# The end of a Fourier transform reordered, two column folds and two low halves moved from GpSimd to VectorE

## The reference

```python
scores = scale * q @ k.T + bias          # causal window of 128, one slope per head
x = softmax(scores) @ v                  # -> (4, 576, 512)
mixed = real(fft(fft(x, axis=1), axis=2))
u = x + mixed
un = (u - mean(u)) / sqrt(var(u) + 1e-6)
x2 = u + relu(un @ w_ch1) @ w_ch2        # 512 -> 2048 -> 512
# gate: one of 8 experts per token, sticky along the sequence
out = p[e] * (relu(x2 @ w1[e]) @ w2[e])  # 512 -> 1024 -> 512
```

## Time and profile before

| | |
|---|---|
| median of 3 runs | 922.79 us |
| lowest, highest | 921.07, 926.31 us |
| profiled execution, its own time | 928.07 us |
| its span, first to last instruction | 926.1 us |
| mean granted TensorE clock | 0.975 of full speed |
| busy: PE, DVE, ACT, POOL | 862.1, 459.1, 316.4, 279.7 us |

### The profile page before, as it was taken

The page is one execution under the profiler, slowest core; times in us unless marked ns, Lnnn a source line. Parts: engine busy times, 40 slices in busy tenths (PEclk is TensorE's granted clock), DMA queues, the critical chain, the costliest instruction groups (busy, mean ns, idle before and its releaser), DMA issues.

```text
span 926.1 us, 22607 instructions
## 1 busy us (share of the span) xinstructions
PE 862.1 (93%) x9091; PEld 623.7 (67%) x9092; DVE 459.1 (50%) x851; ACT 316.4 (34%) x469; POOL 279.7 (30%) x293
## 2 busy tenths in 40 slices
PE   8989897698999999999999999947999999999995
PEld 4767676575676767677777777626767777777773
DVE  6999887557333333342424243748994885000000
ACT  5888886345212111111111111111333333333331
POOL 0467777511020101010101000002444444443332
PEclk9999999899999999999999999968999999999998
DMA  8465533345110101011010102513774773111110
GB/s 285 133 175 173 167 113 108 91 132 183 36 46 23 45 23 45 31 36 44 24 45 24 44 8 67 176 48 95 235 238 153 232 233 115 45 42 45 45 34 0
DMA packets 55608, 88.87 MB, mean 96 GB/s; under 512 B 7148, under 2 KB 26171, under 8 KB 55557
## 3 DMA queue, kind: packets, MB, share of 16 engines
q1 hardware_dynamic: 50117, 72.16, 25.4%
q0 software_dynamic: 5440, 16.00, 5.6%
HBM read 70.80 MB, written 16.55 MB: 94 GB/s over the span
## 4 chain that ended last, share of the span: by engine, by line
PE 72%; DVE 7%; DMA 7%; issue 4%; POOL 3%; ACT 3%; SPq 2%; DVEq 0%; POOLq 0%; ACTq 0%
PE psum L920 19%; PE psum L903 19%; PE psum L1084 13%; PE psum L1100 13%; DMA m_mem<-in_qk 3%; DMA arena<-in_mlp_w 1%; DMA m_mem<-x_rows,m_mem 1%; PE psum L1051 1%; PE psum L655 1%; PE psum L864 1%; DVE m_mem L1404 1%; ACT psum L1159 1%; DVE arena L1425 1%; POOL arena L1880 1%; PE psum L872 1%
## 5 line engine op out<-in xcount | busy, mean ns | idle before, releaser
L903 PE MATMUL psum<-m_mem,arena 128*128 (+1 forms) x1728 | 200.4, 274 | 0.0
L920 PE MATMUL psum<-arena,m_mem 128*128 128x512 f16 x864 | 195.3, 379 | 0.0
L903 PEld LDWEIGHTS psum<-m_mem,arena 128*128 128x128 f16 x1728 | 169.2, 98 | 26.5 <-issue 0.2
L920 PEld LDWEIGHTS psum<-arena,m_mem 128*128 128x128 f16 x864 | 84.5, 98 | 90.4
L1084 PEld LDWEIGHTS psum<-m_mem,arena 128*128 x2400 | 137.3, 97 | 6.9 <-issue 1.5
L1084 PE MATMUL psum<-m_mem,arena 128*128 128x128 f16 x2400 | 139.6, 219 | 1.2 <-issue 0.6
L1100 PE MATMUL psum<-arena,m_mem 128*128 x600 | 133.4, 379 | 0.0
L1270 ACT ACTIVATE m_mem<-psum 128x512 f16<-128x512 f32 x72 | 42.9, 596 | 244.1 <-PE psum L903 244.1
L1100 PEld LDWEIGHTS psum<-arena,m_mem 128*128 128x128 f16 x600 | 57.7, 98 | 65.1
L1965 POOL TENSOR_TENSOR arena<-m_mem,arena 128x1024 f16<-128x1024 f32 x9 | 18.0, 1998 | 271.8 <-ACT arena L1285 226.8
L1591 DVE SCALAR_TENSOR_TENSOR m_mem<-psum,m_mem 128x512 f16<-128x512 f32 x72 | 49.7, 691 | 101.3 <-ACT m_mem L1270 101.2
(11 more groups left out here) (242 smaller groups left out, 1081.7 us busy)
## 6 DMA issues: line engine op xcount, KB each, us to landing
dimdft_sb<-in_exp_w SPq DMA_DIRECT2D x74, 256.0 KB, 3.3
wstage<-in_exp_w SPq DMA_DIRECT2D x54, 256.0 KB, 2.9
m_mem<-in_qk SPq DMA_DIRECT2D x16, 576.0 KB, 4.5
arena<-in_v SPq DMA_DIRECT2D x32, 160.0 KB, 2.7
x_rows<-m_mem SPq DMA_DIRECT2D x16, 320.0 KB, 3.0
x_rows<-arena SPq DMA_DIRECT2D x9, 512.0 KB, 2.8
wstage<-in_mlp_w SPq DMA_DIRECT2D x16, 256.0 KB, 3.4
arena<-in_mlp_w SPq DMA_DIRECT2D x16, 256.0 KB, 3.8
```

The costliest lines, as they stand in the source:

```text
L903: last = nc.tensor.matmul(psum[:, 2 + k % 4, (f % 2) * 2 * P:(f % 2 + 1) * 2 * P], w1_sb[:, sp_, c, f * P:(f + 1) * P], unT[:, bass.ds(t % ...
L920: last = nc.tensor.matmul(psum[:, 6 + q, :], hT[:, k % 4, sp_, at:at + P], w2_sb[:, mp, f, :], start=f == 0 and sp_ == 0 and mp == 0, stop ...
```

## The change

It reorders the instruction lists of all five engines around the end of the transform.

- **SyncE** loads rows 0 to 127 of `x_dram` into `xg[:, 0]` itself (new semaphore `xg0_in`) and issues the load of row 288 of each batch right behind it, after weight chunk 8 and a wait for all stores of x; the latter no longer waits for `ulo_done` 8.
- **TensorE**: `spectrum` waits per chunk for the two pairs of that chunk; transpose_un(0) stands after spectrum(3).
- **ScalarE**: x_hi_of for pairs 12 to 15, the first and second middle rows, the last leftover column and the square root get other places.
- **VectorE** takes fold_d(14) and fold_d(15) (`end_fold_d`) and x_lo_of(14) and x_lo_of(15) (`end_x_lo`); middle_lo_of(2) stands before `normalise_u`, unT_lo_of(0) after spectrum_lo(3).
- **GpSimd** keeps folds and low halves up to pair 13 in another order and gathers only `xg[:, 1]` for tile 0, with row numbers straight from `xrow_sb`. `xg_in` counts 16 less from there on.

```diff
@@ SyncE
-            for n in range(WRING + 2, W_TOP + 3):
+            for n in range(WRING + 2, WRING + 5):
+                load_w(n)
+            for par in range(2):
+                sp.wait_ge(x_stored[par], 16 * PAIRS // 2)
+            sp.dma_start(xg[:, 0, :], x_dram[0:P, :]).then_inc(xg0_in, 16)
+            sp.dma_start(x288[0:B, :], ...[HALF]).then_inc(x288_in, 16)
+            for n in range(WRING + 5, W_TOP + 3):
                 load_w(n)
...
-            for par in range(2):
-                sp.wait_ge(x_stored[par], 16 * PAIRS // 2)
-            sp.wait_ge(ulo_done, DH2 * B)
-            sp.dma_start(x288[0:B, :], ...[HALF]).then_inc(x288_in, 16)
             load_w(W_TOP + 3)
@@ TensorE
-                pe.wait_ge(x_split, PPB * b + PPB)
                 for c in chunks:
+                    pe.wait_ge(x_split, PPB * b + 2 * c + 2)
...
             spectrum(2)
-            transpose_un(0, 4, un_first)
             pe.wait_ge(xl_split, B)
             pe.wait_ge(first_copied, 2)
             middle_rows(B)
             spectrum(3)
+            transpose_un(0, 4, un_first)
@@ ScalarE
-            x_hi_of(PAIRS - 4)
...
             spectrum_hi(0, (0,))
+            x_hi_of(PAIRS - 4)
             x_hi_of(PAIRS - 3)
             spectrum_hi(0, (1,))
+            middle_hi_of(1)
+            spectrum_hi(1, (0,))
+            xl_hi_of(B - 1)
+            spectrum_hi(1, (1,))
             x_hi_of(PAIRS - 2)
-            middle_hi_of(1)
-            x_hi_of(PAIRS - 1)
-            xl_hi_of(B - 1)
-            spectrum_hi(1)
             act.wait_ge(m_clear, 1)
             copy_b(0, first=True, at=4)
-            spectrum_hi(2, (0,))
+            x_hi_of(PAIRS - 1)
+            spectrum_hi(2)
+            middle_hi_of(2)
             std_of(0)
-            spectrum_hi(2, (1,))
+            spectrum_hi(3)
             unT_hi_of(0, at=4)
-            middle_hi_of(2)
-            spectrum_hi(3)
@@ VectorE
             spectrum_lo(1, (0,))
+            def end_fold_d(n):
+                dve.wait_ge(eo_done, PAIRS)
+                dve.wait_ge(ends_copied, B)
+                dve.wait_ge(x_split, n - 1)
+                nc.vector.tensor_tensor(xd[:, n % 2], xb[:, 2, :, 0:P], xb[:, 3, :, P:0:-1],
+                                        ALU.add if n % 2 == 0 else ALU.subtract).then_inc(d_done, 1)
+            def end_x_lo(n):
+                dve.wait_ge(x_hi, n + 1)
+                nc.vector.tensor_tensor(xparts[:, 1, n]..., xd[:, n % 2]..., xparts[:, 0, n]...,
+                                        ALU.subtract).then_inc(x_split, 1)
+            end_fold_d(PAIRS - 2)
             dve.wait_ge(first_ready, 1)
...
             spectrum_lo(1, (1,))
+            end_fold_d(PAIRS - 1)
             fold(0, first=True, at=4)
-            spectrum_lo(2, (0,))
+            for n in range(PAIRS - 2, PAIRS):
+                end_x_lo(n)
+            spectrum_lo(2)
             moments(0)
+            middle_lo_of(2)
             normalise_u(0, un_first)
-            spectrum_lo(2, (1,))
+            spectrum_lo(3)
             unT_lo_of(0, at=4)
-            middle_lo_of(2)
-            spectrum_lo(3)
@@ GpSimd
-            for p in range(PAIRS - 3, PAIRS):
-                fold_x(p)
-                fold_d(p - 1)
-                x_lo_of(p - 2)
-            fold_d(PAIRS - 1)
-            for n in range(PAIRS - 2, PAIRS):
-                x_lo_of(n)
+            fold_x(PAIRS - 3)
+            x_lo_of(PAIRS - 5)
+            fold_d(PAIRS - 4)
+            fold_d(PAIRS - 3)
+            x_lo_of(PAIRS - 4)
+            fold_x(PAIRS - 2)
+            x_lo_of(PAIRS - 3)
+            fold_x(PAIRS - 1)
             xl_lo_of(B - 1)
+            pool.wait_ge(const_in, CONSTS * 16)
+            for par in range(2):
+                pool.wait_ge(x_stored[par], 16 * PAIRS // 2)
+            nc.gpsimd.indirect_dma_start(xg[:, 1, :], None, x_dram[0:B * SP_ROWS],
+                                         bass.IndirectOffsetOnAxis(xrow_sb[:, 0, 1:2], 0)).then_inc(xg_in, 16)
```

More of the change, by code:

```diff
@@ L424, in fused_kernel @@
         xg_in = sem("xg_in")
+        xg0_in = sem("xg0_in")
         ab_ready = sem("ab_ready")
@@ L579, in _ @@
             store_x(PAIRS - 1)
-            for n in range(WRING + 2, W_TOP + 3):
+            for n in range(WRING + 2, WRING + 5):
[3 more added lines that the diff above has]
+            sp.dma_start(xg[:, 0, :], x_dram[0:P, :]).then_inc(xg0_in, 16)
+            sp.dma_start(x288[0:B, :], x_dram[0:B * SP_ROWS, :].rearrange("(b r) d -> r b d", b=B)[HALF])\
+                .then_inc(x288_in, 16)
+            for n in range(WRING + 5, W_TOP + 3):
                 load_w(n)
@@ L592, in load_exp @@
                 sp.dma_start(staging[at], exp_w[m]).then_inc(e_loaded[at], 16)
-            for par in range(2):
-                sp.wait_ge(x_stored[par], 16 * PAIRS // 2)
-            sp.wait_ge(ulo_done, DH2 * B)
-            sp.dma_start(x288[0:B, :], x_dram[0:B * SP_ROWS, :].rearrange("(b r) d -> r b d", b=B)[HALF])\
-                .then_inc(x288_in, 16)
             load_w(W_TOP + 3)
@@ L1555, in fold @@
                 dve.wait_ge(fold_done, 2 * t + 2)
-                dve.wait_ge(xg_in, 32 * t + 32)
+                if first:
+                    dve.wait_ge(xg0_in, 16)
+                else:
+                    dve.wait_ge(xg_in, 32 * t + 16)
                 u = u_of(t, 0)
@@ L1662, in _ @@
             spectrum_lo(1, (0,))
+            def end_fold_d(n):
[6 more added lines that the diff above has]
+                dve.wait_ge(x_hi, n + 1)
+                nc.vector.tensor_tensor(xparts[:, 1, n].rearrange("p t j -> p (t j)"),
+                                        xd[:, n % 2].rearrange("p t j -> p (t j)"),
+                                        xparts[:, 0, n].rearrange("p t j -> p (t j)"), ALU.subtract)\
+                    .then_inc(x_split, 1)
+            end_fold_d(PAIRS - 2)
             dve.wait_ge(first_ready, 1)
@@ L1917, in _, with gather_x @@
                     table_part(p - 1)
-            for p in range(PAIRS - 3, PAIRS):
-                fold_x(p)
-                fold_d(p - 1)
-                x_lo_of(p - 2)
-            fold_d(PAIRS - 1)
-            for n in range(PAIRS - 2, PAIRS):
-                x_lo_of(n)
-            xl_lo_of(B - 1)
-            def gather_x(t, first=False):
-                if not first:
-                    pool.wait_ge(xg_in, 32 * t)
-                    pool.wait_ge(up_done, t)
-                    pool.wait_ge(uq_done, t)
+            fold_x(PAIRS - 3)
[6 more added lines that the diff above has]
+            fold_x(PAIRS - 1)
+            xl_lo_of(B - 1)
+            pool.wait_ge(const_in, CONSTS * 16)
[3 more added lines that the diff above has]
+                                         bass.IndirectOffsetOnAxis(xrow_sb[:, 0, 1:2], 0)).then_inc(xg_in, 16)
+            def gather_x(t):
+                pool.wait_ge(xg_in, 32 * t - 16)
+                pool.wait_ge(up_done, t)
+                pool.wait_ge(uq_done, t)
                 nc.gpsimd.tensor_copy(xidx, xrow_sb[:, bass.ds(t, 1), :].rearrange("p o q -> p (o q)"))\
                     .then_inc(idx_ready, 1)
-                pool.wait_ge(idx_ready, t + 1)
+                pool.wait_ge(idx_ready, t)
                 settle(pool)
                 for q in range(2):
-                    nc.gpsimd.indirect_dma_start(xg[:, q, :], None, x_dram[0:B * SP_ROWS] if first else x_dram,
+                    nc.gpsimd.indirect_dma_start(xg[:, q, :], None, x_dram,
                                                  bass.IndirectOffsetOnAxis(xidx[:, q:q + 1], 0)).then_inc(xg_in, 16)
@@ L1943, in u_q @@
                 pool.wait_ge(fold_done, 2 * t + 2)
-                pool.wait_ge(xg_in, 32 * t + 32)
+                pool.wait_ge(xg_in, 32 * t + 16)
                 if not early:
@@ L1949, in u_q @@
                 nc.gpsimd.tensor_tensor(u[:, FC:D], diff[:, FC - 2:0:-1], xg[:, 1, FC:D], ALU.add).then_inc(uq_done, 1)
-            pool.wait_ge(const_in, CONSTS * 16)
-            for par in range(2):
-                pool.wait_ge(x_stored[par], 16 * PAIRS // 2)
-            gather_x(0, first=True)
-            pool.wait_ge(xg_in, 32)
+            pool.wait_ge(xg_in, 16)
             pool.wait_ge(first_copied, 2)
```

## The result

The changed kernel took **914.68 us** (median of 10 runs, 912.73 to 920.03). The kernel before, run beside it, took 924.74 (10 runs, 921.04 to 926.41), so the ratio is 0.9905 with a 95% interval of 0.9885 to 0.9924: 8.8 us of 924.74, and 7.0 to 10.6 by the interval (the two medians themselves are 10.1 apart). The profiled execution took 914.68 us, its span 912.7.

A forecast was written before the change was run, and what follows sets the result against it. TensorE's gaps between attention and first MLP tile, then VectorE's queue, were taken as the bound. Edge rows stored at 188.7 instead of 197.50 gave 8.8 us, off a median of 922.79: 914.0, range 909.5 to 920.5.

The forecast's parts named there:

- VectorE's queue: VectorE's work from spectrum_lo(1, 1) to unT_lo(0), taken as the bound: 17.9 us, from 169.1 to 187.0.
- The low clock: TensorE at 1.2 GHz for 3.4 us after the first gap, costing 1.7 us in edge and spectrum(1, 1).
- First row: First middle row: ScalarE done at 160.3, VectorE's low half at 162.1, so the first edge starts at 162.25, not 166.26.
- the 167: Sign of being wrong: a granted clock under 1 beyond 167 us.
- rival b: VectorE's queue 3.9 us longer, its instructions with two SBUF inputs meeting GpSimd's work: 917.9 us; chance 0.12.
- the 15.4 us taken from before: VectorE's work from two stretches of the kernel before, 10.88 + 4.52 us; with 2.5 more it made 17.9.
- The 3 us saved is inside the 17.9: Tile 0's transposes moved behind spectrum(3): 3 us saved, counted within VectorE's work and not added again.
- It waits for VectorE, never the other way: TensorE in the seam after 168.2: always waits for VectorE, except once by some tenths for batch 3's last low half.
- The stall before tile 1: TensorE's wait inside tile 0 before tile 1's transposes: hangs on weight loads and stays at about 3.3 us.
- a: Rival: the shortened first gap no longer lowers the clock, 1.7 us come back, 912.3 us; chance 0.11.
- c: Rival: chunk 4 late or ScalarE held, first middle row ready at 164.4, spectrum(1, 1) 3.3 us later: 917.3; chance 0.12.
- e: Rival: several short gaps keep TensorE at 1.2 GHz through the seam, MLP at 201.4, 928.3 us; chance 0.07.

The follow-up runs named there:

- early_again: early_row once more, timed in more rounds on another chip: 910.24 us, ratio 0.9868 to the kernel before.
- row_only: The kernel before, with only ScalarE's first middle row moved ahead of the high half of x pair 14: 924.68 us, ratio 1.0013.
- early_row: The changed kernel with the first middle row earlier on VectorE and ScalarE, and the gate weights split behind the edge rows: 913.86 us, ratio 0.9895.
- gp_keeps: The changed kernel with the last two folds and low halves back on GpSimd, their high halves earlier on ScalarE: 916.64 us, ratio 0.9918.
- dve_more: The changed kernel with two more folds of 640 columns, result unused, on VectorE ahead of its last fold: 917.66 us, ratio 0.9930.
- tab_only: The changed kernel with SyncE's nine routing tables behind the last MLP weight loads: 914.00 us, ratio 0.9902.
- clock_kept: The changed kernel with 16 unused matmuls on TensorE behind spectrum(1, 0), in its gap before the first edge: 915.26 us, ratio 0.9908.

## Why the prediction was right

**The chain held, link by link, and its errors cancelled in part.** Forecast and measured: first `edge` 162.25, 163.52; end of spectrum(1, 1) 168.2, 169.44 (166.29 + 3.15); VectorE's queue starts 169.1, 170.34, and lasts 17.9, 17.0; it ends 187.0, 187.37; edge rows stored 188.7, 189.33; MLP near 187, 187.56. The gain in the seam was 8.2 us for 8.8. The low clock lasted 3.4 us, as forecast, and cost 1.6: 0.9 in `edge` (2.77 for 1.86) and 0.7 in spectrum(1, 1) (3.15 for 2.44). GpSimd's tail ended at 163.0 (near 163), and SyncE's wait cost nothing. The gather landed at 169.0 and not by 168 (5.4 us from its issue, for at most 4.6), under the same cover. That the seam comes out so close is part luck: a first row 1.3 us late and a queue 0.9 short. The 914.0 leans on the 922.79 of three runs besides; the same kernel took 924.74 in ten.

**First row, 1.3 late.** ScalarE was done at 160.28 (160.3 forecast); VectorE was late. I let it be busy until 160, as before; it was busy until 161.19. Of these 1.2 us, 0.5 is that its last products of the attention came later (two weight halves at 151.28 took 2.49 us beside GpSimd, for 1.28 before), and 0.7 is two more halves that took 2.46, for 1.72 before. The rows after stand above; before:

```profile
156.41 1.72 DVE L1453 SCALAR_TENSOR_TENSOR arena<-arena 128x512 f16<-128x512 f32 x2
...
158.70 1.34 DVE L1539 SCALAR_TENSOR_TENSOR wg_sb<-wg_in,wg_sb 128x36 f16<-128x36 f32 x1
```

The gate weights did not make it late, for they cost as much before (1.34, 1.33), but they are held up in the same way. In early_again that instruction has 0.20, with GpSimd idle:

```profile
185.09 0.20 DVE L1717 SCALAR_TENSOR_TENSOR wg_sb<-wg_in,wg_sb 128x36 f16<-128x36 f32 x1
```

That is rival b's mechanism, in a place where I hadn't looked: ahead of the queue. It changes from one execution to the next and not only with the kernel: in row_only, where GpSimd keeps the order of before, the same two halves took 2.94. The late row carried the lower clock to 167.8, past the 167 that I had named as a sign of being wrong. It was one: the whole path up to the queue ran 1.3 us behind the forecast.

**The queue, 0.9 short.** b's contention was there too, and small: L1565 took 0.96 beside GpSimd's L1979, and the same instruction 0.42 in early_row (L1558 there), where GpSimd stood waiting. With the two low halves (2.08 for 2 x 0.78) it makes 1.1 us, for 3.9 in rival b. GpSimd had little left to do, as the forecast said. The sum was long elsewhere: the 15.4 us taken from before held such contention as well. There the two sums of fold 0 took 1.75 us (1.39 after) and a weight half 1.14 (0.67 after). My lower bound for 640 columns, 0.74, doesn't follow from its own terms either: 0.67 and 128 columns at 1.04 ns make 0.80. The 0.83 that I used was right to 0.05.

**The transposes, under-credited.** "The 3 us saved is inside the 17.9" kept the total right and hid what matters: undone, with the order of spectrum(2) as it is, it costs 7.6 us in the seam, since a long gap stands in front of work that then runs at the lower clock. It is not a saving beside the others but what lets them through.

**"It waits for VectorE, never the other way"** was nearly so for the changed kernel: VectorE waits 0.29 us for the second `edge`, which the sum left out, and the edge rows are stored 0.6 late. It fell in gp_keeps: 1.2 us of waiting the other way. TensorE and ScalarE are so close behind that VectorE's work can't be relieved by 2.5 us for a gain of 2.5.

**The stall before tile 1: wrong.** I kept it at 3.3; it was 0.74. In the other profiles tile 0 took 28.1 to 29.8 us, row_only's 29.84 among them, and row_only doesn't beat before. So before's 31.15 belongs at least in part to that one execution. Only two profiles have the old order throughout (31.15 and 29.84, and in both the clock fell after the stall), so it stays open whether the change takes something off tile 0. The medians leave little room for it: 8.8 us less in all, 8.2 of them in the seam. What the stall hangs on, the weight loads as I wrote or VectorE's own work, no run decides.

**Rivals.** a: after the first gap the clock stayed up in dve_more (gap 2.86) and fell in tab_only (2.87), so it is an outcome of some executions rather than of the kernel. c: ScalarE wasn't held, but the row was ready at 163.4, more than half way from 162.1 to c's 164.4, through VectorE. e: the clock recovered after every gap.

## What to carry to other kernels

Count the waits that stand in series on a seam, and forecast them together. Here the first alone gave 0, the first two 2.9 us in the seam, and the third with what goes with it the rest; an experiment that tries one at a time would have dropped the first. So take one part out of the whole as well as putting one into the old kernel: that is what showed the worth of the third. Which engine does a piece of work mattered less than what it stands behind in its queue. When the seam is open, ask what lets the bounding queue start: that gave the next 5 us in the seam, for a few lines moved.

## What the runs showed of the hardware

**A gap lowers the clock in some executions and not in others.** The first gap of the changed kernel and its variants was followed by 3.4 us of the lower level in the changed kernel (gap 3.93), by 6.8 in gp_keeps (4.08; 0.66 in both stretches from 160 to 170), by none in dve_more (2.86; there the next gap, 2.55, was followed by 3.4), and in tab_only (2.87) most of it fell inside the gap (0.71 in 160 to 165, 0.94 in 165 to 170), where it costs nothing. The last `edge`, behind gaps of 1.35 and 1.08 us, ran at the upper level in the changed kernel and at the lower in clock_kept. One such stretch cost 1.6 us in the changed kernel, so one kernel's seam can move by that much between profiles, and differences of that size between two of them aren't read as effects.

**GpSimd and VectorE take turns, instruction by instruction.** In the changed kernel GpSimd's L1979 starts at 173.32 while VectorE's L1564 runs until 173.65, and ends at 174.24: 0.92 us, for the 0.62 that L1984, as wide but on one partition, takes alone. VectorE's L1565 starts at 173.57 and ends at 174.53, 0.29 after L1979. That is about what both would do if each waited for the other's instruction to end (alone, L1565 takes 0.42). The Trainium skill (SBUF — State Buffer, section Who interferes with whom) says that a VectorE instruction with two SBUF inputs and a GpSimd one that reads SBUF exclude each other for a whole instruction; by that rule, the trace agrees. It fits the gate weights as well: an instruction of 0.20 us, which starts 0.12 after L1869 (1.39 us) and ends 0.06 after it, took 1.33. So the price of such contention goes by the length of the other engine's instruction, and a small one pays most for its size.
